# Unit 0's last attention steps placed between the weight joins, x's split and w_out's loads on narrower waits, w_in's pieces ahead of w_out's

## The reference

```python
# attention: q, k, v, f_logit are [4, 8, 768, 48]
f = 1.0 / (1.0 + np.exp(-f_logit))
for t in range(S):
    state = f[:, :, t, :, None] * state + np.einsum('bhd,bhe->bhde', k[:, :, t], v[:, :, t])
    y[:, :, t] = np.einsum('bhd,bhde->bhe', q[:, :, t], state)
x = y.transpose(0, 2, 1, 3).reshape(B * S, H * D)              # [3072, 384]
# first block: w_in [384, 2048], w_out [2048, 384]
h = x @ w_in
g = np.where(h >= 1, h, np.where(h <= -1, 0.0, (h + 1) ** 2 / 4))
x = g @ w_out
# second block: w1, w2 [384, 1024], w3 [1024, 1024], w_out [1024, 384]
out = ((x @ w1) * (x @ w2) @ w3) @ w_out
```

## Time and profile before

| | us |
|---|---|
| median of 3 runs (lowest to highest) | 948.19 (947.43 to 951.37) |
| the profiled execution's own time | 946.54 |
| its span in the trace | 944.6 |
| PE busy in the span | 924.0 (98%) |
| DVE / ACT / POOL busy | 526.3 / 392.5 / 148.6 |

### The profile page before, as it was taken

How to read it: one execution, slowest core, us unless ns; L and a number is a source line. 1 busy time by engine, 2 the same in 40 slices (tenths; PEclk the granted TensorE clock), 3 DMA queues, 4 the chain that set the end, 5 groups by cost and what they waited for, 6 DMA issues and landing times.

```text
span 944.6 us, 24359 instructions
## 1 busy us (share of the span) xinstructions
PE 924.0 (98%) x10722; PEld 860.0 (91%) x10722; DVE 526.3 (56%) x956; ACT 392.5 (42%) x766; POOL 148.6 (16%) x151
## 2 busy tenths in 40 slices
PE   6999799999999999999999999999999999999998
PEld 6989799999999999999999999998888888888887
DVE  6766698767767767768768664463222122213122
ACT  1433555645544644644644544674222222222212
POOL 2414104305205115115125000000000000000000
PEclk9999799999999999999999999999999999999999
DMA  9931820260340430530520200602020202000000
GB/s 267 247 119 43 210 52 2 66 88 2 78 76 2 89 66 2 97 58 1 112 43 2 52 2 2 248 12 93 1 67 1 67 1 68 1 34 0 34 1 34
DMA packets 115834, 57.67 MB, mean 61 GB/s; under 512 B 92433, under 2 KB 111121, under 8 KB 115217
## 3 DMA queue, kind: packets, MB, share of 16 engines
q1 hardware_dynamic: 115728, 56.11, 24.9%
HBM read 45.09 MB, written 11.01 MB: 59 GB/s over the span
## 4 chain that ended last, share of the span: by engine, by line
PE 93%; DVE 5%; DMA 1%; ACT 1%; issue 1%; SPq 0%; DVEq 0%; ACTq 0%
PE bank L1081 16%; PE bank L1083 15%; PE bank L1082 15%; PE bank L1327 11%; PE bank L1326 11%; PE bank L1325 10%; PE bank L1019 4%; PE bank L1056 2%; PE bank L1030 1%; PE bank L1062 1%; PE bank L1043 1%; PE bank L993 1%; DMA first_q<-in_q_dram 1%; PE bank L988 1%; PE bank L998 1%; PE bank L1076 1%
## 5 line engine op out<-in xcount | busy, mean ns | idle before, releaser
L1295 DVE TENSOR_TENSOR product<-bank,a_copy 128x512 f32<-128x512 f32 x48 | 33.2, 692 | 221.1 <-PE bank L1327 221.1
L1081 PE MATMUL bank<-x_hi,w_in_hi 128*128 128x384 f32 x384 | 135.4, 353 | 0.5 <-DVE x_lo L900 0.5
L1081 PE MATMUL bank<-g_hi,w_out_hi 128*128 128x384 f32 x384 | 133.6, 348 | 0.3 <-DVE g_lo L911 0.3
L1083 PE MATMUL bank<-x_hi,w_in_lo 128*128 128x384 f32 x384 | 129.2, 337 | 0.0
L1082 PE MATMUL bank<-x_lo,w_in_hi 128*128 128x384 f32 x384 | 129.0, 336 | 0.0
L1083 PE MATMUL bank<-g_hi,w_out_lo 128*128 128x384 f32 x384 | 128.7, 335 | 0.0
L1082 PE MATMUL bank<-g_lo,w_out_hi 128*128 128x384 f32 x384 | 128.6, 335 | 0.0
L657 ACT ACTIVATE g_hi<-gated 128x384 fp32r<-128x384 f32 x128 | 67.2, 525 | 128.2 <-DVE gated L906 128.2
L1327 PE MATMUL bank<-y_hi,w_lo 128*128 128x512 f32 x288 | 112.8, 392 | 0.0
L1326 PE MATMUL bank<-y_lo,w_hi 128*128 128x512 f32 x288 | 112.7, 391 | 0.0
L1325 PE MATMUL bank<-y_hi,w_hi 128*128 128x512 f32 x288 | 112.0, 389 | 0.0
(11 more groups left out here) (115 smaller groups left out, 1729.7 us busy)
## 6 DMA issues: line engine op xcount, KB each, us to landing
v_leaf<-in_v_dram SPq DMA_DIRECT2D x8, 576.0 KB, 6.5
v_rows<-in_v_dram SPq DMA_DIRECT2D x64, 72.0 KB, 2.7
middle<-middle_out SPq DMA_DIRECT2D x8, 576.0 KB, 3.3
w_rows<-in_moe_w_dram SPq DMA_DIRECT2D x8, 512.0 KB, 10.1
f_leaf<-in_f_logit_dram SPq DMA_DIRECT2D x28, 144.0 KB, 3.8
k_leaf<-in_k_dram SPq DMA_DIRECT2D x28, 144.0 KB, 4.6
q_leaf<-in_q_dram SPq DMA_DIRECT2D x28, 144.0 KB, 4.4
out_dram<-out_rows SPq DMA_DIRECT2D x5, 768.0 KB, 4.0
```

Of the source, the lines that this page charges most:

```text
L1081: nc.tensor.matmul(o, w[0], b[0], start=first, stop=False)
L1083: return nc.tensor.matmul(o, w[1], b[0], start=False, stop=last_)
L1295: nc.vector.tensor_tensor(pf[:, f % RING], b_bank[f % 2][:, 0:GROUP], af[:, f % 2], ALU.mult)\
```

## The change

The steps of unit 0 that stood behind the last join (`y` 1 and 2, `x` 0 to 2, `update` 1) now stand between the joins. The pieces of w_in all precede those of w_out. The stores of the joined product count on two semaphores, four on each. The split of unit 0 waits for the turn that last read its memory, the first high part of g waits for the first four stores, and only the last of the four loads of w_out waits for all stores. `up(0)` and `up(1)` of unit 0 wait for the low parts of the last turned tile. The counts of identity matmuls and all tables of places have other numbers.

```diff
-BEFORE_TURN, BEFORE_JOIN, BEFORE_LEVEL = {0: 40, 1: 12}, 12, (0, 9, 0, 20)
+BEFORE_TURN, BEFORE_JOIN, BEFORE_LEVEL = {0: 40, 1: 16}, 0, (0, 4, 8, 0)
...
-        pieces = halves_in[0:KD] + pairs_out[0:KD] + halves_in[KD:] + pairs_out[KD:]
+        pieces = halves_in + pairs_out
...
-        PIECE_AT = (-8, 6, 18, 28, 29, 30, 31, 33, 33, 36, 39, 43, 43, 44)
+        PIECE_AT = (-6, 7, 14, 23, 24, 24, 32, 33, 34, 35, 35, 41, 41, 41)
...
-                sp.dma_start(w_joined[:, t], joined_rows(t)).then_inc(joined_out, 16)
-            sp.wait_ge(joined_out, 16 * T2)
+                sp.dma_start(w_joined[:, t], joined_rows(t)).then_inc(first_joined_out if t < T2 // 2 else joined_out, 16)
             for n in range(WO_LOADS):
+                if n == WO_LOADS - 1:
+                    sp.wait_ge(first_joined_out, 16 * (T2 // 2))
+                    sp.wait_ge(joined_out, 16 * (T2 // 2))
...
-                    act.wait_ge(joined_out, 16 * T2)
+                    act.wait_ge(turned, 2 * (T2 - 1))
...
+                elif i == 0:
+                    act.wait_ge(first_joined_out, 16 * (T2 // 2))
...
+                elif u == 0:
+                    pe.wait_ge(turned_lo, 2 * (T2 - 1) + i + 1)
```

32 lines of the change are left out of this document (16 added, 16 removed).

## The result

| | before | changed |
|---|---|---|
| median of 15 runs each (lowest to highest), us | 947.0 (945.63 to 951.37) | 952.49 (950.66 to 954.37) |
| the profiled execution's own time, us | 946.54 | 954.35 |
| its span, us | 944.6 | 952.4 |

The ratio is 1.0054, with a 95% interval of 1.0045 to 1.0063: the changed kernel is slower by 5.5 us.

What follows compares the result with a forecast made beforehand. PE bounds the kernel from 311 to 590 us, so only its idle time before 111 us can be won. `up(0)` 7.2 us earlier shrinks to 3.5 at `up(8)`, later units 0: 948.19 - 3.5 = 944.7 us, range 939.5 to 947.7.

Steps and rivals of the forecast that it cites:

- `up(0)` to `up(8)`: First block of unit 0: DVE's eight pieces behind gate 0 make PE wait 5.5 us; `up(8)` at 137.0, lead 3.5.
- `krow` 0 3.2 later as before: End of unit 0's levels: `krow` 0 follows level 3 (55.1) by 3.2 us, at 58.3 instead of 60.41.
- the tightest place stays: Units after unit 0: slack between k_next 1 and level 2 stays 0.64 us, 0.5 between level 3 and krow 0; cost 0.
- The head: Before the first join: w_last's low parts ahead on DVE put `turn` 1 at 29.7 and the join at 31.8, 2.2 us lost.
- The levels: Unit 0, level 0 at 41.1 to `krow` 0 at 58.3: fewer identity matmuls and shorter waits win 4.6 us.
- The moved steps: Steps moved between the joins: 4.1 us more PE work, waits of 1.6, 1.0 and 0.2 us; last join ends at 96.9.
- Last join to `up(0)`: Only six transposing steps remain there, slowed by ACT's copies; `up(0)` at 101.0 instead of 108.2, 7.2 us earlier.
- my walk along PE alone: Behind `up(0)`: 5.5 us of waits added in full to PE's old pace of 32.3, less 0.6, gives `up(8)` at 138.2.
- the middle that I took: `up(8)` at 137.0, between 138.2 from PE's pace with all waits and 136.6 from DVE's own chain.
- Later units: Units after unit 0: same PE work, about two more cut matmul groups per unit at under 0.1 us each; taken as 0.
- my rival for "slower": Later units' tables leave a new wait at krow 0 or before x 2, 1.2 us per unit; 953.1 us, chance 0.08.
- the lead at `up(0)`: How much earlier PE reaches `up(0)` of unit 0: 7.2 us, at 101.0 instead of 108.2.

Runs made afterwards that it cites:

- the first of the four kernels above: The kernel before with only the narrower waits and all of w_in ahead of w_out, all its tables kept: 946.26 us, ratio 0.9995.
- the old head: The changed kernel with unit 0's first steps, w_last's split and the identity matmuls before `turn` 1 and the first join as before: 949.22 us, ratio 1.0020.

## Why the prediction was wrong

| step | forecast | changed kernel, two executions |
|---|---|---|
| `turn` 1 | 29.7 | 31.50, 30.80 |
| level 0 | 41.1 | 42.78, 41.84 |
| level 3 | 55.1 | 56.94, 56.39 |
| krow 0 | 58.3 | 63.79, 60.51 |
| `y` 0 | a wait near 65 | 72.46, 69.16 |
| `up(0)` | 101.0 | 108.37, 104.79 |
| `up(0)` to `up(8)` | 36.0 | 36.90, 36.40 |
| `up(8)` to the first save | +0 | +0.75, +0.74 |
| later units | +0 | +2.2, +2.3 |

Four terms failed. The four low parts of w_last were taken at the 4.2 us that they had before, and took 5.5 to 6.1 beside POOL. "`krow` 0 3.2 later as before" left out the gap inside level 3, and it came 4.1 to 6.9 later. The wait of `y` 2 was taken at 0.2 and was 1.1. And what follows `up(8)` was taken at nothing, with the reason that the tightest place stays, and cost 3.0 us.

**The head.** The order of DVE's work was read rightly, the term was mis-sized: four low parts of w_last at 4.2 us took 6.08. I had the row that showed it and weighed it for the last pieces of w_in, not for the head, where POOL works beside them too. It cost 1.1 to 1.8 us here; the whole changed head cost 3.3 against the old one.

**The levels.** Pitch and filler were right: level 0 to level 3 in 14.2 to 14.6 us where I said 14.0, and the filler that went is worth 4 us. Wrong was "`krow` 0 3.2 later as before". Level 3 to krow 0 took 6.85 and 4.12 us. The gap of 0.7 to 2.1 us inside the level, and the low clock that can follow, I had not thought of; the trace of before has none. Moved out of the level, they gave 3.0 to 3.4 us back. The sum had a slip of its own: its checkpoints (2.2 lost before level 0, `krow` 0 at 58.3 instead of 60.41) give 4.3 won in the levels, not 4.6.

**The moved steps.** Named well: the waits at `y` 0 and update 1 are 1.59 and 1.37 us (forecast 1.6 and 1.0). The one at `y` 2 is 1.14, not 0.2, since I took the state of update 1 to be done sooner. That two of the three can be covered is shown: filling them gave 3.4 to 3.8 us, part of it the clock.

**Last join to `up(0)`.** 4.4 and 4.1 us for a forecast of 4.1. Right. x_lo x3 and the last pieces of w_in ran beside POOL (3.62 us for the three x_lo in the changed kernel) and `up(0)` did not wait for them. DVE's reduction beside POOL kept its 2.54 us. x_lo took 1.00 to 1.39 beside POOL and 0.55 in the kernel before, and in the old head one instruction of POOL, 0.83 us otherwise, took 4.95 while four of DVE's ran. The Trainium skill (SBUF — State Buffer, "Who interferes with whom") says that a reduction never contends with GpSimd, that a tensor_tensor with both inputs in SBUF does, and that the loser is blocked for the whole instruction. These rows agree with it.

**`up(0)` to `up(8)`.** Waits of 1.23 (`down(0)`), 0.69, 1.01, 0.54 and 0.50 us stood where I put 1.1, 1.0, 1.3, 0.6 and 0.7. The forecast of 3.7 us lost was 0.4 to 0.9 short; my walk along PE alone, 37.2, was nearer than the middle that I took. The order of the pieces costs nothing by itself (the first of the four kernels above). That eight of them instead of seven stand behind gate 0, on which I put the blame, no run separates from their places; spread out, the named waits went and others came. And w_out's first load was issued at 105.1, not 98, and landed at about 110.4, which the high part at 114.92 did not wait for. `down(0)` is late as the walk had it: at place 32 the first high part of w_out stands on ACT behind ramp 0, high 0 and ramp 1. At place 31 the wait is gone.

**Later units.** "The tightest place stays" and a cost of 0 was wrong by 2.2 us, and by 0.75 more between `up(8)` and the first save. Of the 2.2, 0.7 come as about 0.1 per unit (all that is left in a kernel with the changed tables and no gap there, that with w_out's old places: 462.84 us), the rest gaps in levels of units 2 and 6. This was my rival for "slower", at a much smaller price; unit 1, inside the first block, is where the same tables cost most, 1.5 us more.

In sum, against the median: the lead at `up(0)` was about 1.6 and not 7.2, a loss of 5.6, and what followed cost 7.1 and not 3.7, another 3.4 (5.1 and 3.9 by the first execution). That is the 9.0 between 3.5 faster and 5.5 slower. Most of what was lost behind `up(0)` is two tables, the steps of unit 1 and later units and the places of w_out's pieces, which must be chosen for each other: with both old, 5.2 us come back.

What stays open: what makes the packet ahead of a gap start late, the loads then under way or something else; and what decides whether the clock falls behind a gap. POOL and DVE at once was not tried by itself.

## What to carry to other kernels

Moving work out of a stall wins what was forecast only if the places of all that shares DVE and ACT behind it fit the new order: here the same move was 5.5 us slower with one set of tables and 6 to 9 faster with the old ones, the old head, two covered waits and the gap moved out of level 3. A table of places is not a sum of edits, so test pairs that share an engine together. And look for idle time without a releaser in dense runs of small matmuls, and for an instruction packet ahead of it in the DMA queues; a few more or fewer instructions in an earlier idle time move it to where it costs less.
